# Loops over blocks in a five-engine kernel: hardware loops in place of unrolled ones

## The chip, the cores and the metric

The kernel runs on one core of one Trainium2 chip. Times are device microseconds (us) of one launch. Everything the reference computes happens in that launch; the host only rearranges inputs beforehand.

## The reference, cut to what matters

Three layers follow each other. The first is a gated recurrent attention over 768 steps for 2 batches of 8 heads of 40 channels; its output, 1536 tokens of 320 channels, goes through two gated feed-forward layers with 1536 hidden channels, the second after a root-mean-square norm.

```python
for t in range(S):
    m_new = np.maximum(f_gate[:, :, t] + m, i_gate[:, :, t])
    f_stab = np.exp(f_gate[:, :, t] + m - m_new)
    i_stab = np.exp(i_gate[:, :, t] - m_new)
    C = f_stab * C + i_stab * outer(v_t, k_t);  n = f_stab * n + i_stab * k_t
    y[:, :, t] = sigmoid(o_gate_t) * (C @ q_t) / max(abs(n @ q_t), 1)
x  = (sigmoid(x @ w_gate) * (x @ w_val)) @ w_out                 # layer 0
xn = x / sqrt(mean(x * x) + 1e-6) * rms_g
y  = (silu(xn @ w_gate2) * (xn @ w_val2)) @ w_out2               # layer 1
```

## The kernel before, in words

The 1536 tokens are cut into NB = 4 blocks of TOK = 384 tokens, and a block into BT = 3 tiles of 128. Each engine has its own instruction stream, written by hand, and the streams meet at counting semaphores.

The attention of block 0 runs first, alone (the order in the table ALONE, pieces "A", "B", "D", "S", "R", "M", "T"). Then come the four blocks of layer 0 and the four blocks of layer 1. While a block of layer 0 is computed, the attention of the next block is woven into it, piece by piece, after each of its 12 hidden chunks and each of its 6 half projections (the table WOVEN); so three of the four layer-0 blocks are woven, and the fourth isn't.

- TensorE (`pe`), L878 on: `layer` runs, per block, `hidden` for 12 chunks f (two halves of 8 matmuls of 384 columns each, L858 to L861, a product split into high and low parts), `project` for three token tiles (L875 to L877), in layer 0 the transposes of the normalised tiles (L757), and at its end it already issues hidden chunk 0 and half of chunk 1 of the block that follows (`after`). `hidden` waits for `hf_done` (L851): chunk f may overwrite the banks of chunk f-2 once VectorE has read them.
- VectorE (`dve`), L690 on: `gate` makes hf (L707) and `h_low` h_lo (L711), and between them stand the attention pieces: `rows` ("A", L546 to L574), the right side of the decay matmul ("B", L644 and L645), `weigh` ("S", L584 and L588) and `combine` ("M", L602 to L621). Small dependent operations are chained by a semaphore of the engine itself, `dve_link`, through `step`.
- ScalarE (`act`) makes sigmoids, exponentials and high parts; GpSimd (`pool`) the reciprocal root of the norm; SyncE (`sp`) issues every DMA.

A block is named by a pair `blk`. Every semaphore value and every slice that depends on it goes through `lin(blk, per, k)` (L58), which gives `per * block + k`. In the kernel before the pair is `(None, b)` with b a Python number, so `lin` gives a number and every loop over blocks is unrolled when the program is built: each engine's stream is one straight line of instructions.

Of the kernel before, what the change touches and what calls it, by code (L numbers as in the profile page):

```python
# [15 lines left out]
BT = 3  # L16
NB = NT // BT
# [38 lines left out]


def lin(blk, per, k=0):  # L58
    return per * blk[1] + k


class StepBuffers:
# [22 lines left out]
def mlstm_moe_kernel(nc, q_t, k_t, k_n, v_n, i_g, f_g, o_g, w_gv, w_o, rms_g, out):  # L85
    ctx = ExitStack()

    def sem(name):
        return ctx.enter_context(nc.semaphore(name))

    with ctx:
# [95 lines left out]
        y_done = sem("y_done")  # L187
# [23 lines left out]
        def bufs(blk, j):  # L211
            return (steps_alone if first(blk) else steps_woven)[j]
# [35 lines left out]
        @block.sync  # L248
        def _(sp):
            def load_rows(a):  # L250
                sp.dma_start(f_r[:, :], f_g[bass.ds(a, 1), :, :].rearrange("n h t -> h (n t)")).then_inc(rows_in, 16)
                sp.dma_start(i_r[:, :], i_g[bass.ds(a, 1), :, :].rearrange("n h t -> h (n t)")).then_inc(rows_in, 16)

            def load_step(blk, j):
                n = lin(blk, BT, j)
                to = bufs(blk, j)

                def of(src):
                    return src[bass.ds(n, 1), :, :]

                for i in range(GH):
                    g1 = sum(h > i for h in HEADS)
                    rs = slice(i * D, (i + 1) * D)
                    sp.dma_start(to.qbd[rs, 0:g1, i * P:(i + 1) * P],
                                 of(q_t)[:, rs, 0:g1 * P].rearrange("n r (g t) -> (n r) g t", t=P)
                                 ).then_inc(step_in[j], 16)
                sp.dma_start(to.kd, of(k_t).rearrange("n r (g t) -> (n r) g t", t=P)).then_inc(step_in[j], 16)
                sp.dma_start(to.qd, of(q_t).rearrange("n r (g t) -> (n r) g t", t=P)).then_inc(step_in[j], 16)
                sp.dma_start(to.va[:, :, 0:D], of(v_n).rearrange("n p (h e) -> (n p) h e", h=H)
                             ).then_inc(step_in[j], 16)  # L270
                sp.dma_start(to.kn, of(k_n).rearrange("n p c -> (n p) c")).then_inc(step_in[j], 16)
                sp.dma_start(to.o_sig, of(o_g).rearrange("n p c -> (n p) c")).then_inc(step_in[j], 16)

            def load_raw(j):
                if j >= RING:
                    wait_split(sp, j - RING)
                src, n = raw_src(j)
                sp.dma_start(raw[:, j % RING, 0:n], src).then_inc(raw_in[j % RING], 16)

            for t in range(BT):  # L280
                sp.sem_inc(out_sent[t], 16)
            load_rows(0)
            for j in range(BT):
                sp.wait_ge(zeroed, j + 1)
                load_step((None, 0), j)
                load_raw(j)
            for j in range(RING, WCH):
                load_raw(j)
            sp.dma_start(g_row[:, :], rms_g.partition_broadcast(P)).then_inc(misc_in, 16)
            for b in range(NB - 1):  # L290
                sp.wait_ge(rows_done, b + 1)
                load_rows(b + 1)

                sp.wait_ge(y_done, lin((None, b + 1), BT))
                load_step((None, b + 1), 0)
                sp.wait_ge(zeroed, BT + 1)
                load_step((None, b + 1), 1)
                sp.wait_ge(y_done, lin((None, b + 1), BT, 1))
                load_step((None, b + 1), 2)

            sp.wait_ge(y_done, BT * (NB - 1) + 2)
            for j in range(WCH, LAYERS * WCH):
                load_raw(j)
            for b in range(NB):
                for t in range(BT):
                    sp.wait_ge(oe_done, BT * b + (NT + t + 1 + 2))
                    sp.dma_start(out[bass.ds(b * TOK + t * P, P), :], y_tok[:, t, 0:DM]).then_inc(out_sent[t], 16)
            for t in range(BT):
                sp.wait_ge(out_sent[t], 16 * (NB + 1))
# [3 lines left out]
        def _(pool):  # L313
# [71 lines left out]
            pool.wait_ge(wo_done, NC)  # L385
            link(pool.memset(in_raw.va[:, :, D:D1], 1.0))
            pool.memset(in_raw.qbd, 0.0).then_inc(zeroed, 1)
            for b in range(NB):
                for t in range(BT):
                    ts = slice(t, t + 1)  # L390
                    pool.wait_ge(ss_done, BT * b + t + 1)
                    pool.tensor_tensor(meansq[:, ts], meansq_in[:, ts], eps[:, :], ALU.add).then_inc(pool_link, 1)  # L392
                    pool.wait_ge(pool_link, BT * b + (links[0] + t + 1))
                    pool.tensor_tensor(rstd[:, ts], meansq[:, ts], half_neg[:, :], ALU.pow).then_inc(rstd_done, 1)  # L394
# [5 lines left out]
        def _(act):  # L400
# [48 lines left out]
            def layer(lay, blk, woven, prepare):  # L449
                def weave(slot):  # L450
                    for what in WOVEN[slot]:
                        piece((blk[0], blk[1] + 1), what, turns(blk, 0))

                def sigmoid(f):
                    n = lin(blk, NF, lay * NB * NF + f)
                    act.wait_ge(g_done, n + 1)
                    act.wait_ge(hf_done, n + 1)
                    act.activation(sg[:, f % 2, :], g_ps[f % 2][:, 0:TOK], ACT.Sigmoid).then_inc(sg_done, 1)  # L458

                def h_high(f):  # L460
                    act.wait_ge(hf_done, lin(blk, NF, lay * NB * NF + f + 1 + 2))
                    if f == 0:
                        act.wait_ge(o_done, lin(blk, BT, lay * NT + 1))
                    act.activation(h_hi[:, f, :], hf[:, f % 2, :], ACT.Copy).then_inc(hhi_done, 1)  # L464

                def x_high(t):
                    act.wait_ge(t_done, turns(blk, t + 1 + 3 + (BT if woven else 0)))
                    act.activation(x_hi[:, :, bass.ds(lin(blk, TOK, t * P), P)], t_view(L_BANK[t]), ACT.Copy).then_inc(xhi_done, 1)

                for f in range(NF):  # L470
                    sigmoid(f)
                    h_high(f)
                    if woven:
                        weave(f)
                    if prepare and f % FC == 0 and f > 0:
                        for j in range(2):
                            high_gv(GVC + 2 * (f // FC - 1) + j)
                if prepare:
                    for j in range(2):
                        high_gv(GVC + GVC - 2 + j)  # L480
                for t in range(BT):
                    n = lin(blk, BT, lay * NT + t)
                    if woven:
                        weave(NF + 2 * t)
                    act.wait_ge(o_done, n + 1 + 1)
                    if lay == 0:

                        act.wait_ge(t_done, turns(blk, (BT if woven else 0) + t + 1))
                        act.activation(y_tok[:, t, 0:DM], o_ps[t][:, 0:DM], ACT.Square, scale=float(DM) ** -0.5,  # L489
                                       accum_out=meansq_in[:, t:t + 1]).then_inc(ss_done, 1)  # L490
                    else:
                        act.wait_ge(out_sent[t], lin(blk, 16, 16))
                        act.activation(y_tok[:, t, 0:DM], o_ps[t][:, 0:DM], ACT.Copy).then_inc(oe_done, 1)
                    if woven:
                        weave(NF + 2 * t + 1)
                if lay == 0:
                    for t in range(BT):
                        x_high(t)

            for b in range(NB - 1):  # L500
                layer(0, (None, b), True, False)
            layer(0, (None, NB - 1), False, True)
            for b in range(NB):
                layer(1, (None, b), False, False)


        @block.vector
        def _(dve):
# [160 lines left out]
            step, k = steps_of((None, 0))  # L669
# [72 lines left out]
                    x_low(turns(blk, turn0 + t), blk, t, L_BANK[t])  # L742
                assert k[0] == (per_block[0] if woven else 0), k

            for b in range(NB - 1):
                layer(0, (None, b), True, False)
            layer(0, (None, NB - 1), False, True)
            for b in range(NB):
                layer(1, (None, b), False, False)


        @block.tensor
        def _(pe):
# [167 lines left out]

            hidden(0, (None, 0), 0)
            hidden(0, (None, 0), 1, (1,))
            for b in range(NB - 1):
                layer(0, (None, b), True, (0, (None, b + 1)))
            layer(0, (None, NB - 1), False, (1, (None, 0)))
            for b in range(NB - 1):
                layer(1, (None, b), False, (1, (None, b + 1)))
            layer(1, (None, NB - 1), False, None)


# [48 lines left out]
```

## Time and profile before

| | us |
|---|---|
| median of three runs | 541.75 |
| lowest and highest | 540.87, 542.2 |
| the profiled execution | 541.75 |
| its span, first to last instruction | 540.0 |
| TensorE busy in the span | 497.2 |
| VectorE busy in the span | 323.4 |
| ScalarE busy in the span | 180.1 |

The profiled execution took as long as the median, and 1.75 us of it lie outside its span. By stretches, the attention of block 0 alone takes the first 73 us, the three woven blocks of layer 0 some 71 us each, the fourth 53 us, and the four blocks of layer 1 about 49 us each. Matmuls are pipelined: their durations overlap, so the distance from one start to the next is what a matmul costs.

### The profile page before, as it was taken

Reading aid. Unit: us, or ns where it says so; the run is one execution under the profiler, and the core shown is the slowest. Engines: PE = TensorE matmul, PEld = TensorE weight load, DVE = VectorE, ACT = ScalarE, POOL = GpSimd, SP = SyncE. Lnnn points to the kernel's source line nnn. Section 1 sums busy time; section 2 is a strip of 40 time slices with the busy share of each in tenths; the row PEclk is TensorE's granted clock in tenths of the full one; section 3 lists DMA queues with packets and bytes.
Section 4 is the critical chain, followed back from the end, with each engine's and each line's share of the span. In section 5 each row is a group of like instructions: output and inputs, shape, how many; then the busy total and the mean of one; then the engine's idle time right before and its main releaser. Section 6 shows DMA issues by size and latency. Waiting matters only on the chain.

```text
span 540.0 us, 7882 instructions
## 1 busy us (share of the span) xinstructions
PE 497.2 (92%) x2948; PEld 474.6 (88%) x2948; DVE 323.4 (60%) x809; ACT 180.1 (33%) x337; POOL 66.3 (12%) x86
## 2 busy tenths in 40 slices
PE   0987169999999999999999999999999999999997
PEld 0755168999998999989999989999999999999997
DVE  7888949787487874788753574575055315513550
ACT  1365013454135540455413553332123213312320
POOL 5275930000100001000010001720000000000000
PEclk9999999999999999999999999999999999999999
DMA  4663341030310202301320233100000000000001
GB/s 121 171 203 122 124 123 30 1 80 1 103 51 2 78 1 63 93 0 41 84 85 1 89 121 122 36 1 1 33 5 1 12 25 2 0 26 13 0 1 36
DMA packets 28869, 28.38 MB, mean 53 GB/s; under 512 B 14240, under 2 KB 25760, under 8 KB 28832
## 3 DMA queue, kind: packets, MB, share of 16 engines
q1 hardware_dynamic: 28832, 27.89, 17.3%
q8 instruction: 23, 0.38, 0.3%
q14 instruction: 14, 0.11, 0.1%
HBM read 25.92 MB, written 1.97 MB: 52 GB/s over the span
## 4 chain that ended last, share of the span: by engine, by line
PE 81%; DVE 14%; issue 2%; ACT 1%; POOL 0%; DVEq 0%; ACTq 0%
PE bank L858 17%; PE bank L859 17%; PE bank L861 11%; PE bank L875 7%; PE bank L877 7%; PE bank L876 7%; PE bank L814 4%; PE bank L797 3%; DVE cst L608 2%; DVE den L615 2%; PE bank L757 2%; PE bank L816 1%; DVE y_tok L618 1%; PE bank L783 1%; DVE wgv_lo L686 1%
## 5 line engine op out<-in xcount | busy, mean ns | idle before, releaser
L858 PE MATMUL bank<-x_hi,wgv_hi 128*128 128x384 f32 x576 | 199.2, 346 | 2.3 <-DVE x_lo L626 1.2
L859 PE MATMUL bank<-x_lo,wgv_hi 128*128 128x384 f32 x576 | 193.6, 336 | 0.0
L861 PE MATMUL bank<-x_hi,wgv_lo 128*128 128x384 f32 x384 | 129.2, 336 | 0.0
L858 PEld LDWEIGHTS bank<-x_hi,wgv_hi 128*128 128x128 f32 x576 | 108.9, 189 | 4.7 <-DVE wgv_hi L687 1.7
L859 PEld LDWEIGHTS bank<-x_lo,wgv_hi 128*128 128x128 f32 x576 | 109.0, 189 | 1.4
L464 ACT ACTIVATE h_hi<-hf 128x384 fp32r<-128x384 f32 x96 | 50.4, 525 | 151.6 <-DVE hf L707 151.6
L875 PE MATMUL bank<-wo_hi,h_hi 128*128 128x320 f32 x288 | 91.9, 319 | 0.5 <-DVE hf L707 0.5
L877 PE MATMUL bank<-wo_hi,h_lo 128*128 128x320 f32 x288 | 89.0, 309 | 0.0
L876 PE MATMUL bank<-wo_lo,h_hi 128*128 128x320 f32 x288 | 89.0, 309 | 0.0
L705 DVE TENSOR_TENSOR sg<-sg,bank 128x384 f32<-128x384 f32 x48 | 26.6, 554 | 98.1 <-PE bank L859 90.4
L861 PEld LDWEIGHTS bank<-x_hi,wgv_lo 128*128 128x128 f32 x384 | 72.6, 189 | 0.0
L707 DVE TENSOR_TENSOR hf<-sg,bank 128x384 f32<-128x384 f32 x96 | 53.1, 553 | 27.7 <-PE bank L859 17.4
L458 ACT ACTIVATE sg<-bank 128x384 f32<-128x384 f32 x96 | 46.2, 481 | 33.8 <-PE bank L859 33.0
L711 DVE TENSOR_TENSOR h_lo<-hf,h_hi 128x384 fp32r<-128x384 f32 x96 | 55.9, 583 | 0.6
L875 PEld LDWEIGHTS bank<-wo_hi,h_hi 128*128 128x128 f32 x288 | 54.1, 188 | 1.7 <-DVE hf L707 0.8
L876 PEld LDWEIGHTS bank<-wo_lo,h_hi 128*128 128x128 f32 x288 | 54.1, 188 | 0.9
L877 PEld LDWEIGHTS bank<-wo_hi,h_lo 128*128 128x128 f32 x288 | 54.1, 188 | 0.0
L392 POOL TENSOR_TENSOR meansq<-meansq_in,eps 128x1 f32<-128x1 f32 x12 | 2.3, 189 | 259.5 <-ACT y_tok L489 259.5
L735 DVE SCALAR_TENSOR_TENSOR y_tok<-bank,rstd,g_row 128x320 f32<-128x320 f32 x12 | 6.6, 552 | 35.0 <-POOL rstd L394 35.0
L757 PE MATMUL bank<-ident,y_tok 128*128 128x128 f32 x72 | 13.0, 293 | 14.6 <-DVE y_tok L621 14.6
L757 PEld LDWEIGHTS bank<-ident,y_tok 128*128 128x128 f32 x72 | 9.7, 149 | 17.6 <-DVE y_tok L621 17.1
L489 ACT ACTIVATE y_tok<-bank 128x320 f32<-128x320 f32 x12 | 5.3, 438 | 54.8 <-PE bank L877 54.8
(143 smaller groups left out, 563.8 us busy)
## 6 DMA issues: line engine op xcount, KB each, us to landing
raw<-in_w_gv SPq DMA_DIRECT2D x16, 576.0 KB, 4.1
raw<-in_w_o SPq DMA_DIRECT2D x8, 480.0 KB, 3.3
y<-y_tok SPq DMA_DIRECT2D x12, 160.0 KB, 1.8
step_a<-in_k_t SPq DMA_DIRECT2D x7, 180.0 KB
step_a<-in_q_t SPq DMA_DIRECT2D x7, 180.0 KB
step_a<-in_v_n SPq DMA_DIRECT2D x7, 160.0 KB
step_a<-in_k_n SPq DMA_DIRECT2D x7, 160.0 KB
step_a<-in_o_g SPq DMA_DIRECT2D x7, 160.0 KB
```

The costliest lines, as they stand in the source:

```text
L458: act.activation(sg[:, f % 2, :], g_ps[f % 2][:, 0:TOK], ACT.Sigmoid).then_inc(sg_done, 1)
L464: act.activation(h_hi[:, f, :], hf[:, f % 2, :], ACT.Copy).then_inc(hhi_done, 1)
L705: dve.tensor_tensor(sg[:, u, :], sg[:, u, :], g_ps[u][:, 0:TOK], ALU.mult).then_inc(silu_done, 1)
L707: dve.tensor_tensor(hf[:, u, :], sg[:, u, :], v_ps[u][:, 0:TOK], ALU.mult).then_inc(hf_done, 1)
L711: dve.tensor_tensor(h_lo[:, f, :], hf[:, f % 2, :], h_hi[:, f, :].bitcast(F32), ALU.subtract).then_inc(h_done, 1)
L757: mm = pe.transpose(t_view(ps)[:, k, :], y_tok[:, slot, k * P:(k + 1) * P], ident[:, :])
L858: pe.matmul(ps[:, 0:TOK], wgv_hi[:, w, k, cs], x_hi[:, k, xs], start=(k == 0), stop=False)
L859: mm = pe.matmul(ps[:, 0:TOK], wgv_hi[:, w, k, cs], x_lo[:, k, xs], start=False, stop=(k == 2))
L861: pe.matmul(ps[:, 0:TOK], wgv_lo[:, w, k, cs], x_hi[:, k, xs], start=False, stop=False)
L875: pe.matmul(ps, h_hi[:, f, ts], wo_hi[:, f, :], start=(f == 0), stop=False)
L876: pe.matmul(ps, h_hi[:, f, ts], wo_lo[:, f, :], start=False, stop=False)
L877: mm = pe.matmul(ps, h_lo[:, f, ts], wo_hi[:, f, :], start=False, stop=(f == NF - 1))
```

## The change

Nine loops over blocks become hardware loops, each on the engine that runs it: two on SyncE, one on GpSimd, two on ScalarE, two on VectorE and two on TensorE. The body is in the program once and ends with a register addition and a compare-and-branch that jumps back to its first instruction. The pair becomes `(b, k)` with b a register, and `lin` returns an expression `per * reg + (per * off + k)`; semaphore values that were constants are computed into registers, and slices of x_hi, x_lo, kb, nb, the inputs and the output that were constants take their offset from a register. What is computed is the same, and so is the order of the arithmetic instructions on each engine. On TensorE the loop of layer 0 runs blocks 0 to 2 (the fourth is still written out) and the loop of layer 1 blocks 0 to 2; ScalarE and VectorE loop over blocks 0 to 2 of layer 0 and over all four of layer 1.

```diff
 def lin(blk, per, k=0):
-    return per * blk[1] + k
+
+    reg, off = blk
+    return per * off + k if reg is None else per * reg + (per * off + k)
...
-            for b in range(NB - 1):
+            with sp.Fori(0, NB - 1) as b:
                 sp.wait_ge(rows_done, b + 1)
                 load_rows(b + 1)
 
-                sp.wait_ge(y_done, lin((None, b + 1), BT))
-                load_step((None, b + 1), 0)
+                sp.wait_ge(y_done, lin((b, 1), BT))
+                load_step((b, 1), 0)
...
-            for b in range(NB):
+            with sp.Fori(0, NB) as b:
                 for t in range(BT):
                     sp.wait_ge(oe_done, BT * b + (NT + t + 1 + 2))
...
-            for b in range(NB):
+            with pool.Fori(0, NB) as b:
...
-            for b in range(NB - 1):
-                layer(0, (None, b), True, False)
+            with act.Fori(0, NB - 1) as b:
+                layer(0, (b, 0), True, False)
             layer(0, (None, NB - 1), False, True)
-            for b in range(NB):
-                layer(1, (None, b), False, False)
+            with act.Fori(0, NB) as b:
+                layer(1, (b, 0), False, False)
...
-            for b in range(NB - 1):
-                layer(0, (None, b), True, False)
+            with dve.Fori(0, NB - 1) as b:
+                layer(0, (b, 0), True, False)
             layer(0, (None, NB - 1), False, True)
-            for b in range(NB):
-                layer(1, (None, b), False, False)
+            with dve.Fori(0, NB) as b:
+                layer(1, (b, 0), False, False)
...
-            for b in range(NB - 1):
-                layer(0, (None, b), True, (0, (None, b + 1)))
+            with pe.Fori(0, NB - 1) as b:
+                layer(0, (b, 0), True, (0, (b, 1)))
             layer(0, (None, NB - 1), False, (1, (None, 0)))
-            for b in range(NB - 1):
-                layer(1, (None, b), False, (1, (None, b + 1)))
+            with pe.Fori(0, NB - 1) as b:
+                layer(1, (b, 0), False, (1, (b, 1)))
             layer(1, (None, NB - 1), False, None)
```

Lines of the changed kernel stand two further down than the same lines before. VectorE, from a `combine` to the next `weigh` in a woven block. Before:

```order
L615 SCALAR_TENSOR_TENSOR den<-num,den 128x2 [waits dve_link]
L616 RECIPROCAL rden<-den 128x2 [waits dve_link]
L618 TENSOR_TENSOR y_tok<-inter,rden 128x80 [waits t_done,dve_link]
L621 COPY y_tok<-y_tok 128x64 [waits dve_link]
L644 CAST d_lhs<-hl 40x128 [waits d_done,rows_done]
L645 TENSOR_TENSOR d_rhs<-hl,sel 40x1024
L584 TENSOR_TENSOR vk<-raw,wexp 128x328 [waits exp_done,step_in1]
L588 TENSOR_TENSOR wexp<-bank,wexp 128x384 [waits s_done,vk_done]
```

The same place on VectorE in the changed kernel:

```order
L617 SCALAR_TENSOR_TENSOR den<-num,den 128x2 [waits dve_link]
L664 REGISTER_ALU
L618 RECIPROCAL rden<-den 128x2 [waits dve_link]
L664 REGISTER_ALU
L620 TENSOR_TENSOR y_tok<-inter,rden 128x80 [waits t_done,dve_link]
L664 REGISTER_ALU
L623 COPY y_tok<-y_tok 128x64 [waits dve_link]
L645 REGISTER_ALU [waits rows_done]
L646 CAST d_lhs<-hl 40x128 [waits d_done]
L647 TENSOR_TENSOR d_rhs<-hl,sel 40x1024
L586 TENSOR_TENSOR vk<-raw,wexp 128x328 [waits exp_done,step_in1]
L588 REGISTER_ALU
```

The arithmetic is in the same order; a register addition stands ahead of each wait whose value depends on the block, and one of them (L645) holds a wait itself. The layer-0 body has on VectorE 300 instructions, of them 100 register additions and 14 fused groups of register operations.

On TensorE the end of the layer-0 loop and what it jumps to. The last rows of the changed kernel's layer-0 body on TensorE:

```order
L863 MATMUL bank<-x_hi,wgv_lo 128x384
L860 MATMUL bank<-x_hi,wgv_hi 128x384
L861 MATMUL bank<-x_lo,wgv_hi 128x384
L926 REGISTER_ALU
L926 COMPARE_AND_BRANCH
```

And its first rows, to which the branch goes back:

```order
L926 ISA
L853 ISA [waits oe_done]
L860 ISA [waits hf_done]
L860 MATMUL bank<-x_hi,wgv_hi 128x384
L861 REGISTER_ALU
L861 MATMUL bank<-x_lo,wgv_hi 128x384
```

ISA is a fused group of register operations. Before, the next block's matmuls followed directly. TensorE's layer-0 body has 385 matmuls in the built program (437 pairs of weight load and matmul once the compiler has split the plain float32 ones) and 80 other instructions; its layer-1 body has 300 matmuls and 37 others. ScalarE's bodies have 105 and 62 instructions, VectorE's 300 and 74, GpSimd's 14, SyncE's 43 and 11. None of the loops announces its backward branch ahead of time.

## Rows read from the trace of the kernel before

**Rows 1.** The page: span, busy time, granted clock in 40 slices.
```profile
span 540.0 us, 7882 instructions
...
PE 497.2 (92%) x2948; PEld 474.6 (88%) x2948; DVE 323.4 (60%) x809; ACT 180.1 (33%) x337; POOL 66.3 (12%) x86
...
PEclk9999999999999999999999999999999999999999
```

**Rows 2.** Busy time by stretch: one woven block of layer 0, one block of layer 1.
```profile
core 0: us, PE busy (x) PEld busy (x) DVE busy (x) ACT busy (x) POOL busy (x), PEclk, DMA share, GB/s
139.20:210.10 70.90, 69.73 (x439) 65.86 (x438) 51.56 (x157) 28.36 (x53) 2.22 (x6) 1.00 0.17 45
389.50:438.70 49.20, 49.20 (x303) 49.20 (x302) 19.03 (x36) 12.39 (x27) 0.00 (x0) 1.00 0.03 11
```

**Rows 3.** TensorE's sequencer (PEldq) at one wait of `hidden`, layer 0, 217 to 219 us.
```profile
engine op xcount: duration ns min/median/max, first and last start us, forms
L851 PEldq EVENT_SEMAPHORE  x1: 51/51/51, 218.4 to 218.4; - x1
```

**Rows 4.** Timeline of that seam: start us, us, engine, line, tiles [idle before].
```profile
219.81 0.49 ACT L468 ACTIVATE x_hi<-bank 128x384 fp32r<-128x384 f32 x1 [1.23 <-PE bank L757]
...
220.20 0.48 ACT L458 ACTIVATE sg<-bank 128x384 f32<-128x384 f32 x1
...
220.33 0.56 DVE L626 TENSOR_TENSOR x_lo<-bank,x_hi 128x384 fp32r<-128x384 f32 x1 [1.17 <-ACT x_hi L468]
...
220.81 0.55 DVE L707 TENSOR_TENSOR hf<-sg,bank 128x384 f32<-128x384 f32 x1
...
221.02 0.33 PE L858 MATMUL bank<-x_hi,wgv_hi 128*128 128x384 f32 x1
221.20 0.33 PE L859 MATMUL bank<-x_lo,wgv_hi 128*128 128x384 f32 x1
...
223.19 0.55 DVE L707 TENSOR_TENSOR hf<-sg,bank 128x384 f32<-128x384 f32 x1 [0.55 <-ACT sg L458]
```

**Rows 5.** The same sequencer wait, layer 1, 390 to 391 us.
```profile
L851 PEldq EVENT_SEMAPHORE  x1: 51/51/51, 390.8 to 390.8; - x1
```

**Rows 6.** TensorE's timeline at the layer-1 seam.
```profile
389.68 0.34 PE L858 MATMUL bank<-x_hi,wgv_hi 128*128 128x384 f32 x1
...
393.87 0.33 PE L858 MATMUL bank<-x_hi,wgv_hi 128*128 128x384 f32 x1
```

**Rows 7.** The page: DMA queues (packets, MB, share of 16 engines); output issues, landing us.
```profile
q8 instruction: 23, 0.38, 0.3%
q14 instruction: 14, 0.11, 0.1%
...
raw<-in_w_gv SPq DMA_DIRECT2D x16, 576.0 KB, 4.1
...
y<-y_tok SPq DMA_DIRECT2D x12, 160.0 KB, 1.8
```

**Rows 8.** VectorE's sequencer: the 13 semaphore increments at its start.
```profile
L521 DVEq EVENT_SEMAPHORE  x13: 21/21/21, 0.8 to 1.9; - x13
```

**Rows 9.** Timeline of VectorE between two gates of a woven block.
```profile
171.62 0.16 DVE L615 SCALAR_TENSOR_TENSOR den<-num,den 128x3 f32<-128x3 f32 x1
171.82 0.18 DVE L616 RECIPROCAL rden<-den 128x3 f32<-128x3 f32 x1
172.03 0.28 DVE L618 TENSOR_TENSOR y_tok<-inter,rden 128x120 f32<-128x120 f32 x1
172.34 0.56 DVE L588 TENSOR_TENSOR wexp<-bank,wexp 128x384 f32<-128x384 f32 x1
173.40 0.56 DVE L707 TENSOR_TENSOR hf<-sg,bank 128x384 f32<-128x384 f32 x1 [0.50 <-PE bank L859]
```

**Rows 10.** Timelines where TensorE meets a `weigh` and the decay's right side.
```profile
163.67 0.50 PE L783 MATMUL bank<-d_rhs,d_lhs 128*128 128x512 f32 x1 [0.71 <-DVE d_rhs L645]
...
173.26 0.75 PEld L814 LDWEIGHTS bank<-step_a,wexp 128*128 128x128 f32 x6
...
182.73 0.56 DVE L588 TENSOR_TENSOR wexp<-bank,wexp 128x384 f32<-128x384 f32 x1
...
183.35 0.74 PEld L814 LDWEIGHTS bank<-raw,wexp 128*128 128x128 f32 x6 [0.20 <-DVE wexp L588]
```

**Rows 11.** TensorE's sequencer: two waits with eight pairs between them (215 to 217 us).
```profile
L851 PEldq EVENT_SEMAPHORE  x1: 51/51/51, 215.4 to 215.4; - x1
...
L898 PEldq EVENT_SEMAPHORE  x1: 51/51/51, 216.4 to 216.4; - x1
```

More of the change, by code:

```diff
@@ L289, in _ @@
             sp.dma_start(g_row[:, :], rms_g.partition_broadcast(P)).then_inc(misc_in, 16)
-            for b in range(NB - 1):
+            with sp.Fori(0, NB - 1) as b:
                 sp.wait_ge(rows_done, b + 1)
                 load_rows(b + 1)
-                sp.wait_ge(y_done, lin((None, b + 1), BT))
-                load_step((None, b + 1), 0)
+                sp.wait_ge(y_done, lin((b, 1), BT))
+                load_step((b, 1), 0)
                 sp.wait_ge(zeroed, BT + 1)
-                load_step((None, b + 1), 1)
-                sp.wait_ge(y_done, lin((None, b + 1), BT, 1))
-                load_step((None, b + 1), 2)
+                load_step((b, 1), 1)
+                sp.wait_ge(y_done, lin((b, 1), BT, 1))
+                load_step((b, 1), 2)
             sp.wait_ge(y_done, BT * (NB - 1) + 2)
```

## The prediction, made before the changed kernel was run

> **What bounds the kernel now.** I read the page first, then busy time by stretch, then the waits and timelines at the places where the new branches will stand. The page says that TensorE is busy 92% of the span at the full granted clock [rows 1]. By stretch it is tighter: in a woven block of layer 0 it is busy 69.73 of 70.90 us, in a block of layer 1 49.20 of 49.20 [rows 2]. So after the first 73 us the end is set by TensorE, and nothing that other engines gain can show. The change takes no arithmetic away and shortens no matmul. It can only cost, where it makes TensorE stop, or cost nothing. VectorE matters in layer 0 alone: 51.56 of 70.90 us busy there, 19.03 of 49.20 in layer 1 [rows 2]. The span is 540.0 us, and 1.75 us lie outside it, so the profiled execution is 541.75, the median; I add to that.
>
> How far TensorE's instruction reader (its sequencer) is ahead of its array decides what a stop of the reader costs. In layer 0 it handles the wait of hidden chunk 1 at 218.4 us [rows 3]. That chunk's first matmul starts at 221.02 [rows 4]. The lead is 2.6 us. At the same seam of layer 1 it is 390.8 [rows 5] against 393.87 [rows 6], 3.1 us. These waits stand just behind the place of the new branch, so the reader can stop for 2.6 or 3.1 us before the array notices. The lead is regained quickly: eight pairs of load and matmul lie between the reader's waits at 215.4 and 216.4 [rows 11], 0.12 us a pair, while the array starts a matmul each 0.18 us (221.02 to 221.20) [rows 4].
>
> **What a backward branch costs its own engine.** The trace of before has none. Instructions arrive by DMA: 23 packets for TensorE's stream, 0.38 MB, so 16 KB each, and 14 for the other engines, 8 KB each [rows 7]. With 2948 loads and 2948 matmuls [rows 1] that is about 256 instructions a packet on TensorE; the other four have about 1800 in the program, so 128 a packet. TensorE's layer-0 body of about 950 instructions is 3.7 packets, its layer-1 body of about 640 is 2.5, VectorE's layer-0 body of 300 is 2.3; the other bodies are under one packet, but may straddle two. If the first packet of the body is gone when the branch is taken, it must come again. Lower bound: 0.1 us, the price of an instruction that the sequencer handles alone (13 of them from 0.8 to 1.9 us, 0.09 each) [rows 8]. Upper bound: 4.1 us, issue to landing of the 576 KB weight load; the nearest row is the 160 KB output store at 1.8 us [rows 7], to which the packet's own time is to be added. That time is 0.3% of 16 times 540 us over 23 packets, 1.1 us on TensorE, and 0.1% over 14, 0.6 us, elsewhere [rows 7]. That makes 2.9 and 2.4; I take 3.0 us for both, since landing and restart are in neither row.
>
> [...]
>
> **Seam of layer 0, taken twice.** VectorE's last step of a body is x_lo at 220.33, and the gate of the next block comes at 220.81 [rows 4]. The branch is read right after x_lo starts. With 3.0 us for the packet and 0.3 for one addition and the fused group and wait at the body's head (three times 0.1), gate 0 starts 3.3 us late. In the kernel before VectorE waits 0.55 us ahead of the second gate at 223.19 [rows 4]; that much is absorbed. From there to the right side of the decay matmul it has no idle time worth the name, and TensorE already waits for that: 0.71 us at 163.67 [rows 10]. So the rest reaches TensorE: 3.3 - 0.55 = 2.75 us. ScalarE branches at the same moment, after x_hi at 219.81 and ahead of sg at 220.20 [rows 4]; if its body is gone too, both wait side by side. TensorE's own branch costs 3.0 + 0.5 (addition, branch, three fused groups) - 2.6 of lead = 0.9, inside the 2.75. Two taken branches (three blocks in the loop): **5.5 us**, between 0 and 2 x (4.1 + 0.3 - 0.55) = 7.7.
>
> **Seam of layer 1, taken twice on TensorE.** 3.0 + 0.5 - 3.1 = 0.4 us each, **0.8 us**; between 0 and 2 x 1.5 = 3. VectorE's and ScalarE's layer-1 branches hide: VectorE is done with a block at its last h_lo, before the projections, and is busy 19.03 of 49.20 us [rows 2].
>
> **Register operations inside the bodies.** VectorE gets 100 additions and 14 fused groups per woven block, at 0.09 us (rows 8's price of a sequencer-only instruction; no row shows an addition). Most are covered: one that stands between two dependent operations is read while the first runs. RECIPROCAL starts 0.20 us after the operation ahead of it and y_tok 0.21 after that [rows 9], longer than 0.09. Exposed are those that themselves hold a wait, since the next operation can be issued only after them; there are 23 in the body, about 5 in the stretch up to the decay's right side and two or three at each turn from one unit to the next. They reach TensorE only where it waits for VectorE. For most `weigh` steps there is slack: the one that starts at 172.34 and takes 0.56 [rows 9] ends at 172.90, and TensorE's loads start at 173.26 [rows 10]. In three of nine units a block there is none: weigh ends at 183.29 and the loads start at 183.35 [rows 10]. So per woven block 5 x 0.1 + 3 x 0.25 = 1.25 us, and three blocks make **3.75 us**, between 0 and 9 (if a fused group or a wait on a register costs three times as much, and the 0.36 us of slack is used up).
>
> TensorE's 43 additions and 11 groups per block (4 to 5 us of sequencer time) fit in the difference between 0.18 and 0.12 us a pair. SyncE and GpSimd have their deadlines far off: GpSimd's body is 14 instructions, SyncE's loads are issued tens of us ahead. The unwoven fourth block and the start are as before.
>
> **Sum:** 5.5 + 0.8 + 3.75 = 10.05 us; 541.75 + 10.05 = **551.8 us**, 1.9% slower.
>
> **The rivals.** *All bodies stay resident* (the other side). The branch decides at one point: whether the head of the body is still in the engine's instruction memory. If it is, a branch costs about 0.1 us, VectorE's delay at the seam is 0.4, under the 0.55 it idles there, and TensorE's 0.6 lies under its lead of 2.6. Then only the register terms are left, 0 to 3.75 us: 541.75 to 545.5. It isn't slower when the waits on registers hide as well, that is when the exposed share per woven block is under 0.5 us; then the time is 541.75 to 543.4. For it: TensorE's stream is bigger than any other's and fetched in larger pieces. Against: TensorE's 23 packets are as many as its whole stream crosses [rows 1, 7], so in the kernel before each piece was fetched while the stream ran on, and nothing shows that an old one is kept. 20%, of which half counts as no change.
>
> *TensorE becomes bound by its sequencer.* Each hidden half has 8 matmuls whose moving operand takes its address from a register, 192 in a body, 1152 in six passes through TensorE's two bodies. The free rate is 0.12 us a pair and the array's 0.18 [rows 4, 11], so up to 0.05 to 0.06 us more per matmul is free. If a register address costs 0.09 us, the price of a wait [rows 8], each pair takes 0.21 against 0.174 by the hidden matmuls' spacing (24 pairs from 389.68 to 393.87 [rows 6]), and 1152 x 0.036 = 41 us are added: 593 us. Against: the address is read by the same instruction, not by one more. 10%.
>
> *The register operations cost more than a wait does.* With 0.2 us each, the exposed 1.25 us a block become 2.5, and the six `weigh` steps with slack 0.36 [rows 9, 10] lose some 0.15 us each: 3.4 us a block, 10.2 in all, and with the seams 16.5: 558 us. 20%, up to 566.
>
> *Faster.* Nothing TensorE waits for is removed; fewer packets to fetch is worth nothing to an engine that is busy all the time. 3%.
>
> **How the numbers follow.** The forecast, 547 to 556 us, has 47%; more costly register operations or fetches, to 566, 20%; resident bodies 20%; sequencer-bound 10%; faster 3%. The range takes the first two and the slower three quarters of the resident case: 543 to 566 us. A measurement of this kernel tells 0.3%, 1.6 us, from no change. Faster by more 3%, within 10%, slower 87%.
>
> **What would show it.** Right: at the two seams of layer 0 (near 150 and 221 us, the latter moved by the first) a gap of about 3 us on VectorE between x_lo and the next gate that no semaphore explains, more instruction packets than before on both instruction queues per instruction executed, and TensorE waiting 1.7 to 3.5 us for the decay's right side or the first hf. Resident: VectorE's gap under 0.5 us. Sequencer-bound: hidden matmuls farther apart than 0.174 us in the middle of a chunk. Register term: woven blocks longer than 70.9 us by about 1.25 apart from the seam; layer-1 blocks 49.2 us apart from the seam. Wrong altogether: a layer-1 block that grows by microseconds in its middle.

## The result, and the profile after

| | before | changed |
|---|---|---|
| median, us | 541.98 | 558.32 |
| lowest and highest, us | 540.87, 542.69 | 557.16, 559.02 |
| runs | 4 | 4 |

The changed kernel takes 1.0299 times as long, 95% interval 1.0281 to 1.0317: 16.3 us more. The forecast was 551.8 us in a range of 543 to 566; within it, 547 to 556 us was held most likely (47%), and the measured time lies above that.

The page of the changed kernel, the lines that answer to [rows 1] and [rows 7] (the last two: queue, packets, MB, share of 16 engines):

```profile
span 556.6 us, 8903 instructions
...
PE 502.4 (90%) x2948; PEld 478.7 (86%) x2948; DVE 323.0 (58%) x809; ACT 180.3 (32%) x337; POOL 66.6 (12%) x86
...
PEclk9997579999979999989999999999999999999999
...
q8 instruction: 12, 0.20, 0.1%
q14 instruction: 19, 0.16, 0.1%
```

VectorE, ScalarE and GpSimd are as busy as before. TensorE is busy 5.2 us longer with the same matmuls, and the other 11 us or so of the longer span are idle time. TensorE's instruction packets fell from 23 to 12, those of the other engines rose from 14 to 19, though they too execute from a shorter program. And the granted TensorE clock, 9 in every slice before, dips at three places. The first, from 50 to 77 us, lies ahead of the seams, and nothing is lost there (see the last section); the other two are at the seams. By stretch the loss is easy to find (in these rows the third figure from the end is the granted clock). The first two rows are the changed kernel's second woven block (from the last projection of one block to that of the next) and a block of layer 1, columns as in [rows 2]:

```profile
139.51:218.97 79.46, 72.69 (x440) 68.34 (x439) 51.53 (x157) 28.47 (x53) 2.23 (x6) 0.96 0.15 40
```
```profile
406.00:455.14 49.14, 49.14 (x303) 49.14 (x301) 19.02 (x36) 12.39 (x27) 0.00 (x0) 1.00 0.03 10
```

The woven block grew from 70.90 to 79.46 us, the layer-1 block not at all (49.20 and 49.14 us, [rows 2]). So nothing is lost in layer 1. In layer 0 the loss stands at the seam. VectorE's timeline there, and its sequencer's own instructions at the loop's line (count, durations in ns, first and last start in us). `<-issue` marks idle time in which the engine waited for nothing that the profile shows:

```profile
149.97 0.56 DVE L628 TENSOR_TENSOR x_lo<-bank,x_hi 128x384 f32 x1 [1.17 <-ACT x_hi L470]
156.46 0.56 DVE L709 TENSOR_TENSOR hf<-sg,bank 128x384 f32<-128x384 f32 x1 [5.94 <-issue]
```
```profile
L747 DVEq ALU_OP  x1: 40/40/40, 150.0 to 150.0; - x1
L747 DVEq COMPARE_BRANCH  x1: 63/63/63, 150.1 to 150.1; - x1
L747 DVEq FUSED_REGOPS  x1: 63/63/63, 154.1 to 154.1; - x1
```

Before, the gate's start came 0.48 us after that of x_lo (220.33 and 220.81, [rows 4]); now it is 6.49 us. The branch is read at 150.1, the body's first instruction at 154.1: 4.0 us. Then, with nothing but one semaphore wait between, the gate starts at 156.46: another 2.4 us. Two stops one behind the other, where I had counted one of 3.0. TensorE's own branch, and ScalarE's, at the same seam:

```profile
L926 PEldq COMPARE_BRANCH  x1: 238/238/238, 148.0 to 148.0; - x1
L926 PEldq FUSED_REGOPS  x1: 50/50/50, 148.3 to 148.3; - x1
```
```profile
L502 ACTq COMPARE_BRANCH  x1: 45/45/45, 149.4 to 149.4; - x1
L502 ACTq FUSED_REGOPS  x1: 50/50/50, 149.7 to 149.7; - x1
```

They cost 0.3 us each. Of these three, only VectorE's branch stops. TensorE's timeline shows the price of that, and a second one:

```profile
151.66 0.34 PE L861 MATMUL bank<-x_lo,wgv_hi 128*128 x1
157.07 0.69 PE L860 MATMUL bank<-x_hi,wgv_hi 128*128 x1 [5.07 <-DVE hf L709]
157.56 0.53 PE L861 MATMUL bank<-x_lo,wgv_hi 128*128 x1
157.88 0.53 PE L863 MATMUL bank<-x_hi,wgv_lo 128*128 x1
...
162.36 0.43 PE L860 MATMUL bank<-x_hi,wgv_hi 128*128 x1
162.63 0.34 PE L861 MATMUL bank<-x_lo,wgv_hi 128*128 x1
162.80 0.33 PE L863 MATMUL bank<-x_hi,wgv_lo 128*128 x1
```
```profile
151.00:157.00 6.00, 1.00 (x6) 0.68 (x4) 0.54 (x2) 0.00 (x0) 0.00 (x0) 0.89 0.19 58
157.00:162.30 5.30, 5.23 (x16) 5.23 (x17) 3.40 (x9) 1.92 (x4) 0.00 (x0) 0.50 0.00 2
162.40:166.00 3.60, 3.60 (x22) 3.60 (x21) 2.94 (x8) 1.02 (x2) 0.00 (x0) 0.98 0.00 0
```

TensorE waits 5.07 us for the first hf. When it starts again its granted clock is 0.50 for the next 5.3 us: 16 matmuls start 0.32 us apart where the next ones start 0.17 apart. That costs 16 x (0.32 - 0.174) = 2.3 us more. The seam's bill is 5.07 + 2.3 and some smaller losses behind it; the block grew by 79.46 - 70.90 = 8.6 us.

### The profile page after: what moved, and what is told of

Same layout as the page of the kernel before. It is cut to its first block, busy times and chain, and to the rows that moved or that the text cites. A ratio compares the mean times of both kernels' runs of the same rounds, so it can differ in the third digit from the quotient of the medians.

```text
span 556.6 us, 8903 instructions
## 1 busy us (share of the span) xinstructions
PE 502.4 (90%) x2948; PEld 478.7 (86%) x2948; DVE 323.0 (58%) x809; ACT 180.3 (32%) x337; POOL 66.6 (12%) x86
## 3 DMA queue, kind: packets, MB, share of 16 engines
q1 hardware_dynamic: 28832, 27.89, 16.9%
## 4 chain that ended last, share of the span: by engine, by line
PE 46%; issue 40%; DVE 7%; POOL 4%; ACT 1%; POOLq 0%; DVEq 0%; ACTq 0%
PE bank L860 10%; PE bank L861 10%; PE bank L863 7%; PE bank L877 5%; PE bank L878 5%; PE bank L879 5%; POOL wo_lo L378 2%; DVE wgv_lo L688 1%; PE bank L816 1%; ACT wgv_hi L411 1%; POOL wo_hi L376 1%; PE bank L799 1%; POOL wgv_lo L362 1%; DVE hf L709 1%; DVE cst L610 1%
## 5 line engine op out<-in xcount | busy, mean ns | idle before, releaser
L860 PE MATMUL bank<-x_hi,wgv_hi 128*128 (+1 forms) x576 | 202.0, 351 | 11.9 <-DVE hf L709 10.7
L861 PE MATMUL bank<-x_lo,wgv_hi 128*128 (+1 forms) x576 | 195.9, 340 | 0.0
L863 PE MATMUL bank<-x_hi,wgv_lo 128*128 (+1 forms) x384 | 130.8, 341 | 0.0
L860 PEld LDWEIGHTS bank<-x_hi,wgv_hi 128*128 128x128 f32 x576 | 110.9, 192 | 14.9 <-DVE hf L709 10.2
L861 PEld LDWEIGHTS bank<-x_lo,wgv_hi 128*128 128x128 f32 x576 | 110.9, 193 | 1.4
L863 PEld LDWEIGHTS bank<-x_hi,wgv_lo 128*128 128x128 f32 x384 | 73.8, 192 | 0.0
L759 PE MATMUL bank<-ident,y_tok 128*128 128x128 f32 x72 | 12.6, 286 | 14.5 <-DVE y_tok L623 14.5
```

The source lines that it names most:

```text
L759: mm = pe.transpose(t_view(ps)[:, k, :], y_tok[:, slot, k * P:(k + 1) * P], ident[:, :])
L860: pe.matmul(ps[:, 0:TOK], wgv_hi[:, w, k, cs], x_hi[:, k, xs], start=(k == 0), stop=False)
L861: mm = pe.matmul(ps[:, 0:TOK], wgv_hi[:, w, k, cs], x_lo[:, k, xs], start=False, stop=(k == 2))
L863: pe.matmul(ps[:, 0:TOK], wgv_lo[:, w, k, cs], x_hi[:, k, xs], start=False, stop=False)
```

## The experiments

My theory after the comparison: VectorE's layer-0 branch, taken twice, makes the whole loss. Its body doesn't stay in the engine's instruction memory, and TensorE pays for the stop twice, by waiting and by a lower clock. Rivals: register operations and register addresses on all engines (A); TensorE's own branch (B); a branch that drains the engine instead of fetching (C). ("Fetch" means that a packet of instructions comes by DMA.)

### One loop undone

```diff
-            with dve.Fori(0, NB - 1) as b:
-                layer(0, (b, 0), True, False)
+            for b in range(NB - 1):
+                layer(0, (None, b), True, False)
```

> The changed kernel with one loop undone: VectorE's layer-0 loop is written out again, all other eight loops stay. Theory (the loss is VectorE's backward branch, taken twice, whose packets must come again, and what TensorE loses by waiting for it): the time falls by 16 us to 541.5 to 543.5 us, both seams of layer 0 cost nothing, and the TensorE clock stays at 1.00. Rival A (register operations and register addresses on all engines share the loss): with VectorE's 100 additions a block gone but TensorE's and ScalarE's left, 545 to 552 us. Rival B (TensorE's own backward branch is what hurts): no change, 557 to 559 us.

Measured: 542.06 us, ratio to the kernel before 1.0003 (0.9993 to 1.0013). The other eight hardware loops, TensorE's with 1152 register-addressed matmuls among them, cost nothing that can be measured. From the matmul that starts at 80.02 us in the trace of before to the one at 300.15, a stretch with nearly all of the loop in it, TensorE takes 220.14 us here against 220.13. Rival B falls, and rival A for every engine but VectorE: this run takes away VectorE's branch and its register operations together. The run with the body at place 0, below, keeps those operations, and the same stretch takes 221.08 us, so they are worth 0.95 us. (I had expected a granted clock of 1.00; in the profiled execution it is 0.959, but see the last section: it was low up to 75 us, ahead of the seams.)

### That loop alone

The kernel before, with `lin` as changed and VectorE's layer-0 loop as `dve.Fori`; nothing else.

> The kernel before with one part of the change: only VectorE's layer-0 loop is a hardware loop, everything else is written out. Theory: this alone makes the whole loss, 556 to 560 us, with two gaps of 5 to 6 us on VectorE between x_lo and the next gate, and a granted TensorE clock near 0.96. The place of the body in the instruction packets is the same as in the changed kernel, since all that stands ahead of it on VectorE is the same. Rival A: about a third to a half of the loss, 546 to 550 us. Rival B: 542 to 543 us.

Measured: 556.22 us, ratio 1.0274 (1.0257 to 1.0291). This one loop makes some 14.5 of the 16.3 us. The waits of that run (us in total, times, longest) show the stops a little shorter than in the changed kernel, whose longest is 5.9:

```profile
DVE hf L709 <- issue: 10.2, 2, 5.3
PE bank L860 <- DVE hf L709: 9.4, 4, 4.4
```

In the two profiled executions the difference is 3.2 us, and all of it lies at the two seams: TensorE waits 9.4 us for hf in place of 10.7, and runs at half clock for a shorter time behind each wait (at the first seam 2.9 us in place of 5.3). What sets the length of a packet's way, 4.0 us at one seam of the changed kernel and 3.5 at the other, stays open. SyncE's loads of the attention inputs run at the same moment (0.49 MB between 150.1 and 158 us); no run moved them.

### The branch announced

```diff
-            with dve.Fori(0, NB - 1) as b:
+            with nc.Fori(0, NB - 1, engines=[mybir.EngineType.DVE], hint_back_edge=True) as b:
```

The changed kernel, with one instruction more in VectorE's layer-0 loop: at the head of each pass stands the announcement of the backward branch (BRANCH_PREFETCH_HINT in the trace, three times, 39 to 56 ns of VectorE's sequencer).

> [...] Theory (the stall is a fetch): the gap of 4.0 us between the branch and the first instruction of the body falls under 1 us; the second fetch, three instructions into the body, may stay with 2.3 us. Without the second 542 to 544 us; with it, VectorE is 2.3 us late, TensorE waits 1 to 2 us at each seam: 544 to 549 us. Rival C (the gap isn't a fetch, the branch drains or restarts the engine): no change, 557 to 559 us.

Measured: 542.79 us, ratio 1.0024 (1.0014 to 1.0034). Both stops are gone, not only the first, and the run fetches 9 packets on the queue of the engines other than TensorE. The result told less than it seemed: one instruction more at the head can also place the body differently, so it was repeated below with the place held.

### The body at the beginning of a packet

```diff
-            with dve.Fori(0, NB - 1) as b:
+            with nc.Fori(0, NB - 1, engines=[mybir.EngineType.DVE], head_slot={mybir.EngineType.DVE: 0}) as b:
```

`head_slot` asks for the place of the body's first instruction; this run's trace, below, shows what the places count from.

> The changed kernel with VectorE's layer-0 body placed so that its first instruction is the first of a packet; nothing else moves. Theory (two fetches one after the other, 4.0 us for the branch target and 2.3 us three instructions later, because the body begins at the very end of a packet): the second gap disappears, the first stays. The gate comes 2.3 us earlier at both seams: TensorE waits about 2.8 us in place of 5.1, and the time is 558.3 minus 4.6, 553.7 us, or 549 to 551 us if the shorter wait also spares the fall of the clock. Rival C: no change, 557 to 559 us.

Measured: 542.22 us, ratio 1.0014 (1.0003 to 1.0024). My expectation was wrong: I thought that the second stop would go and the first stay, and both went. VectorE at the seam and its sequencer:

```profile
149.37 0.56 DVE L628 TENSOR_TENSOR x_lo<-bank,x_hi 128x384 f32 x1 [1.18 <-ACT x_hi L470]
150.04 0.56 DVE L709 TENSOR_TENSOR hf<-sg,bank 128x384 f32<-128x384 f32 x1
```
```profile
L747 DVEq COMPARE_BRANCH  x1: 69/69/69, 149.5 to 149.5; - x1
L747 DVEq FUSED_REGOPS  x1: 63/63/63, 149.8 to 149.8; - x1
```

The branch takes 0.3 us, and the whole run fetches 9 packets on that queue, in place of 19:

```profile
q14 instruction: 9, 0.07, 0.0%
```

In the loop's first pass the body's instructions 129 and 257 start at 108.4 and 134.5 us, and a packet comes on that queue at 109.0 and at 135.3. So the places count from a packet's beginning, and a packet holds 128 instructions.

The body is the same 300 instructions, register operations included. So it isn't its length alone that loses it. Beginning at a packet's first place it touches three packets. In the changed kernel the second stop comes ahead of the body's third instruction, which suggests that the body begins at a packet's very end and touches four. That gave theory D: VectorE keeps four packets of 128 and always loads one ahead; a body that touches three stays whole, one that touches four loses its first when the fifth is loaded. Its rivals: the head must stand at a packet's beginning (E), or something coarser than the packet border counts, such as the distance from it (F). The next four runs test them.

### Four places for the same body

The same edit with other places: 72, 84, 86 and 100. A body of 300 instructions that begins at place 84 ends with its third packet (84 + 300 = 384 = 3 x 128).

> The changed kernel, VectorE's layer-0 body of 300 instructions placed with its first instruction at place 72 of a packet of 128: it touches three packets (72 + 300 = 372, under 384). Theory D (the engine keeps four packets of 128, one of them loaded ahead, so a body that touches three stays resident and one that touches four, as the changed kernel's, loses its first): no packet comes again at the seams, 541.5 to 543 us. Rival E (the head must stand at a packet's beginning): a fetch at each branch, gaps of about 4 us on VectorE, 548 to 554 us.

> The same with the first instruction at place 100: the body touches four packets (100 + 300 = 400, over 384), with 28 instructions ahead of the next packet's beginning. Theory D: the branch waits about 3.5 to 4 us for its packet at both seams, and the packet behind it comes while 28 instructions run or is late as well by up to 2.3 us; TensorE waits 2.5 to 5 us at each seam, 547 to 558 us. Theory D': one fetch alone, TensorE waits 2.8 us, and the clock doesn't fall: 547 to 548 us. Rival E: as place 72, whatever that is.

> The changed kernel, VectorE's layer-0 body with its first instruction at place 84 of a packet of 128: its last of 300 is then the last of the third packet (84 + 300 = 384). Theory D (a body that touches three packets of four stays): 541.5 to 543 us, no packet at the seams. Rival F (what counts is something coarser than the packet border, the distance of the head from it, say): some value between those of places 72 and 100, 542 to 551 us, in either run of this pair alike.

> The same two instructions later, place 86: the register addition and the branch at the body's end stand in a fourth packet. Theory D: as at place 100, a fetch of the head's packet at both seams, 548 to 553 us, 8 us more than at place 84 for a shift of two instructions. Rival F: the same time as at place 84.

| first instruction at place | packets touched | us | ratio to before (95%) |
|---|---|---|---|
| 0 | 3 | 542.22 | 1.0014 (1.0003 to 1.0024) |
| 72 | 3 | 542.10 | 1.0012 (1.0001 to 1.0023) |
| 84 | 3 | 542.82 | 1.0025 (1.0015 to 1.0034) |
| 86 | 4 | 554.16 | 1.0234 (1.0205 to 1.0262) |
| 100 | 4 | 550.57 | 1.0166 (1.0146 to 1.0186) |

Two instructions' shift, from 84 to 86, costs 11.3 us. Rivals E and F fall, and theory D stands. The border is shown by these times. That it is a packet's is shown in the first pass at place 84: the instructions counted as the first of the second and third packet, the body's 45th and 173rd, start at 89.4 and 118.2 us, and packets come at 89.8 and 118.8. The loading ahead is shown by the packets: with the body at place 100 five come in one pass of the loop (149 to 224 us), with the body at place 84 none (149 to 222 us).

```profile
q14 instruction: 5, 0.04, 0.2%
```

They start at 151.2, 153.6, 159.8, 192.0 and 215.3 us. Counted from place 100, the instructions that begin the body's second, third and fourth packet start at 159.5, 190.3 and 216.3 us. So the next packet comes, within 2 us, as one is entered, and after a stop at the branch the whole body comes again, not its first packet alone. That four are kept is the reading that makes three stay and four not; no run shows the memory itself. At place 100 the stop at the branch can be seen alone, without the second stop:

```profile
149.01 0.56 DVE L628 TENSOR_TENSOR x_lo<-bank,x_hi 128x384 f32 x1 [1.17 <-ACT x_hi L470]
153.23 0.55 DVE L709 TENSOR_TENSOR hf<-sg,bank 128x384 f32<-128x384 f32 x1 [3.65 <-issue]
```
```profile
L747 DVEq COMPARE_BRANCH  x1: 69/69/69, 149.1 to 149.1; - x1
L747 DVEq FUSED_REGOPS  x1: 63/63/63, 153.0 to 153.0; - x1
```

The branch waits 3.9 us for the target's packet; the next packet's arrival is hidden by the 28 instructions ahead of its border. TensorE waits 2.8 us. I had expected 547 to 548 us for that case with the clock unmoved, or up to 558 with both stops. It was 550.6. In the profiled execution, 552.25 us, the clock fell after this shorter wait too (0.60 from 155 to 158 us). That isn't all of it: one of the four executions had a mean granted clock of 1.00 and still took 550.24 us, and it left no trace that would say where.

### Fetch or placement: the announcement at place 100

> As the run at place 100, with the backward branch announced at the head of each pass. In the earlier run with the announcement the body could have been placed anew as well, so that it didn't tell the fetch from the placement; here the place is held. Theory (the stall is the fetch of the target's packet, and the announcement brings it before the branch): gap at the branch under 1 us, 542 to 545 us. Rival C (it was the placement): as the run at place 100 without it.

(What this expectation calls rival C is the placement, not the draining branch of the earlier ones.)

```diff
-            with dve.Fori(0, NB - 1) as b:
+            with nc.Fori(0, NB - 1, engines=[mybir.EngineType.DVE], head_slot={mybir.EngineType.DVE: 100}, hint_back_edge=True) as b:
```

Measured: 542.33 us, ratio 1.0023 (1.0011 to 1.0034), against 550.57 at the same place without it.

```profile
L747 DVEq COMPARE_BRANCH  x1: 92/92/92, 148.6 to 148.6; - x1
L747 DVEq BRANCH_PREFETCH_HINT  x1: 39/39/39, 148.9 to 148.9; - x1
L747 DVEq FUSED_REGOPS  x1: 63/63/63, 149.0 to 149.0; - x1
```

```profile
q14 instruction: 10, 0.08, 0.0%
```

The placement is held and the stop is gone, 0.4 us from branch to body. The run fetches 10 packets where place 100 without the announcement fetches 20, so the fetches are not hidden but left out. The placement as the cause falls, and so does the draining branch: the same branch from the same place costs 0.4 us once the fetches are gone. How the announcement keeps the body in place isn't shown by any run.

### The same stop without a branch

The kernel before, with dependent copies on VectorE at the two seams, 24 in one run and 12 in the other:

```diff
+                if b < NB - 2:
+                    for n in range(24):
+                        dve.tensor_scalar(inter[:, :, :], num[:, :, :], 1.0, None, ALU.mult).then_inc(stalled, 1)
+                        dve.wait_ge(stalled, 24 * b + n + 1)
```

> The kernel before, with no hardware loop, and 24 dependent copies of a small tile added on VectorE at the two places where the changed kernel branches (the copies write a scratch tile, nothing else changes). They hold VectorE for some 5 to 7 us. Theory (it is the length of VectorE's stop that costs, and TensorE's clock falls by waiting, whatever the cause): TensorE waits the stop less about 0.9 us, its clock falls to half for about 5 us after it, and each seam costs the stop plus 1.5 to 2.5 us: 553 to 560 us. Rival (the clock falls by something the branch itself does): each seam costs the stop less 0.55 us and the clock stays at 1.00 there, 551 to 554 us.

> The kernel before, no hardware loop, with 12 dependent copies of a small tile on VectorE at the two seams in place of 24 (a scratch tile is written, nothing else changes): VectorE is held 3.1 us. Theory (the length of the stop sets the price): TensorE waits about 2.0 us at each seam, its clock falls less long or not at all, and the whole costs 2 x (3.1 - 0.55) = 5.1 us, up to 7 with the clock: 546 to 549 us. Rival (a stop costs the same whatever its length, through the clock): 551 us or more.

Measured: 554.87 us (1.0248, 1.0223 to 1.0272) with 24 copies, 547.05 us (1.0104, 1.0084 to 1.0125) with 12. The waits of the two runs (total, times, longest):

```profile
PE bank L863 <- DVE hf L708: 11.2, 4, 5.0
```
```profile
PE bank L863 <- DVE hf L708: 5.0, 4, 2.0
```

The clock, in the run with 24 copies while TensorE waits, after it, and later; then in the run with 12 copies at the same place:

```profile
150.90:155.90 5.00, 0.06 (x1) 0.00 (x0) 4.38 (x20) 0.00 (x0) 0.00 (x0) 0.97 0.04 12
156.00:158.70 2.70, 2.70 (x8) 2.70 (x9) 2.60 (x5) 1.40 (x3) 0.00 (x0) 0.50 0.00 0
158.80:161.00 2.20, 2.20 (x14) 2.20 (x13) 1.01 (x3) 0.49 (x1) 0.00 (x0) 0.95 0.00 0
```
```profile
155.00:158.00 3.00, 3.00 (x20) 3.00 (x19) 2.90 (x8) 1.59 (x4) 0.00 (x0) 1.00 0.00 0
```

A wait of 5.0 us behind ordinary copies takes TensorE to half its clock, as the branch did; it is the wait that does it, not the branch. It stays there for 2.7 us here and for 5.3 at the changed kernel's seam, after waits of the same length, so this term isn't a fixed price: 1.2 us here (8 matmuls) and 2.3 there.

With 12 copies the two seams differ, though TensorE waits 1.95 us at both. At the first the clock stays at 1.00 (the row above). At the second it falls:

```profile
226.35 0.57 PE L863 MATMUL bank<-x_hi,wgv_hi 128*128 128x384 f32 x1 [1.95 <-DVE hf L708]
```
```profile
226.80:230.00 3.20, 3.20 (x12) 3.20 (x11) 2.96 (x6) 1.45 (x4) 0.00 (x0) 0.51 0.01 3
230.20:232.00 1.80, 1.80 (x12) 1.80 (x11) 0.83 (x2) 0.24 (x1) 0.00 (x0) 1.00 0.00 0
```

So a stop of 3.1 us on VectorE costs 2.2 us where the clock holds and 3.8 us where it falls; the run's 5.9 us (547.05 less 541.16) are these two together. These runs don't give a length of wait below which the clock is safe.

## Why the prediction held, and where its steps were off

Lying in the range was worth less than it looks: the sum came out 6 us short, and two terms erred in opposite directions. What each seam cost can be read by following the same matmuls through the traces. In the trace of before, the first seam lies between the matmuls that start at 148.18 and 160.14 us, the second between those at 218.06 and 232.12, and the stretch from 80.02 to 300.15 holds nearly all of layer 0's loop. How much longer than before each took, in us:

| kernel | first seam | second seam | rest of the stretch | together |
|---|---|---|---|---|
| changed | 7.9 | 7.1 | 1.9 | 16.9 |
| VectorE's loop alone | 6.0 | 5.8 | 1.9 | 13.7 |
| body at place 100 | 4.7 | 5.9 | 0.9 | 11.4 |
| body at place 86 | 5.4 | 6.7 | 0.5 | 12.7 |
| body at place 0 | 0.0 | 0.0 | 1.0 | 1.0 |
| before, 24 copies | 6.7 | 7.1 | -0.2 | 13.6 |
| before, 12 copies | 2.2 | 3.8 | -0.2 | 5.9 |

- **What bounds the kernel, and which engine matters at which seam:** right. TensorE is busy without a gap in layer 1, nothing was lost there, and in layer 0 VectorE's delay arrives at TensorE nearly whole.
- **Seam of layer 0,** 2.75 us each: mis-sized. It measured 7.9 and 7.1 us, where even the bound for both together was 7.7. The packet took 4.0 and 3.5 us, inside the bounds of 0.1 and 4.1, where I took 3.0 (the output store's landing plus the packet's own time was the nearest row). The second packet, 2.4 us at the first seam, was missing from the sum: I counted packets per body and not where the body begins. And the fall of the clock, 2.3 us, was missing too. No row of before could show it, since its clock is 9 in every slice of [rows 1], but nowhere does its TensorE stop for 5 us in the steady part either; the bound had to be left open upward.
- **VectorE's idle time ahead of the second gate,** 0.55 us, was the wrong slack. TensorE stops earlier on the path than the sum had it, at the first hf. It waits 5.07 us there for a gate that comes 6.0 us later (6.49 less 0.48), and 2.8 us at place 100 for one that comes 3.7 later. So 0.9 us is absorbed before TensorE needs hf.
- **Seam of layer 1,** 0.8 us: nothing (49.14 us a block). The lead of 3.1 us wasn't even needed, since TensorE's packets didn't come again: between 147 and 320 us, where it takes its layer-0 branch twice, its queue brings none. A body of 950 instructions, 3.7 of its packets, stays resident; so of my two readings the "resident" rival was right for TensorE and ScalarE and the fetch right for VectorE. On VectorE the border lies at a packet of 8 KB and 128 instructions (542.8 us at place 84, 554.2 at 86). TensorE's branch goes back over 3.7 packets of 16 KB without a fetch, and no run here looks for the length at which its body would be lost.
- **Register operations,** 3.75 us in three blocks: 0.95 us, where the body stays whole (221.08 less 220.13; 0.9 to 1.0 also at places 72 and 84 and in both announced runs). With its body at place 0 the second woven block takes 71.38 us against 70.90:

```profile
138.90:210.28 71.38, 69.88 (x439) 65.86 (x438) 51.54 (x157) 28.28 (x53) 2.23 (x6) 1.00 0.16 44
```

  An addition takes 0.08 us of VectorE's sequencer from one instruction to the next, not far from the 0.09 I used; the mistake was to call five of them exposed at the front of the block: at place 0 the stretch of the first seam, 148.18 to 160.14 before, isn't longer at all. In the changed kernel the rest of the stretch is 1.9 us longer and not 0.95; the reason was not followed up.
- **Sequencer-bound TensorE:** rightly kept small. The hidden matmuls still start 0.17 us apart.

The measured terms are 7.9 + 7.1 + 1.9 = 16.9 us, less 0.4 us that the start of the changed kernel's profiled execution gained: 16.5 us (16.3 by the medians). They are read from the result, so they are an account and not a test. The measured 558 us also stood in the prediction, under a rival, dearer register operations, and that rival was wrong in its mechanism: the slow end of the range held for a reason that the prediction didn't have.

None of the versions beats the kernel before; the one with all nine loops and VectorE's body at place 0 or 72 comes within 0.15% of it.

## What to carry to other kernels

Before a loop body goes onto hardware, count for each engine how many instruction packets it touches, begin and end included, not only how long it is: for two branches, 300 instructions on VectorE cost about 1 us in three packets and 10 to 16 us in four, and both a chosen place for the head and an announced branch repair it. Find the engine whose lead at the seam is smallest, because there a stop arrives nearly whole. TensorE's lead of 2.6 to 3.1 us would not have hidden a fetch of 3.5 to 4.0 us either, had it needed one; it was saved by keeping its body. When a stop makes TensorE wait for about two microseconds or more, allow for matmuls that it will then run at half clock: 1.2 to 2.3 us at a seam here, and nothing at one of the two seams with the shortest wait.

## What the runs showed of the hardware that was not expected

- VectorE's border lies between a body that ends with its third packet (542.8 us) and one that reaches two instructions into the fourth (554.2 us). Above it the whole body is fetched again in every pass, five packets a pass with the one loaded ahead.
- With the branch announced, the body that touches four packets is not fetched again either: 10 packets in the run and 542.33 us at place 100.
- The granted clock over a whole run says little here. The run at place 84 has a mean of 0.956 and is 1.7 us above before, of which 1.0 us is the register term. Executions of the kernel before, too, have means from 0.956 to 1.00. At place 84 the clock was low up to 79 us alone, and in the first 70 TensorE waits for others half of the time:

```profile
0.00:70.00 70.00, 35.85 (x125) 27.52 (x125) 60.12 (x143) 22.45 (x28) 42.36 (x52) 0.72 0.48 143
70.00:80.00 10.00, 7.88 (x28) 7.48 (x29) 2.64 (x7) 1.51 (x3) 1.77 (x3) 0.57 0.42 117
80.00:541.00 461.00, 453.17 (x2797) 439.85 (x2795) 260.59 (x661) 156.03 (x306) 22.16 (x32) 1.00 0.12 37
```

- Place 86 costs 3.6 us more than place 100 by the medians and 1.5 us by the profiled executions, though both touch four packets; its TensorE waits up to 3.7 us against 2.8. Packets on the queue from 149 to 156 us, first at place 86, then at place 100:

```profile
q14 instruction: 3, 0.02, 1.5%
```
```profile
q14 instruction: 2, 0.02, 0.8%
```

  At place 86 VectorE enters its fourth packet with the last two instructions of the body. The fetch of the packet behind it (150.9 us) is then just under way when the head's is fetched (151.4 us), and the stop at the branch takes 4.3 us in place of 3.9. No run tests this reading of the times.
